# Whole pieces on TensorE in the layer tiles, and an earlier start of the first expert slot

## The chip, the core and the metric

One core of a Trainium2 chip runs the whole program in one launch. The metric is device time in microseconds (us); a run is compared with others of the same kernel on the same kind of core.

## The reference, cut to what matters

The program computes three layers on 4 x 768 = 3072 tokens with 8 heads of 48.

1. A scan with complex decay: for each head `S = a * S + k v^T` and `y = q S` (real part), with `a` scaled to a magnitude of at most 0.999.
2. `h = x @ w_in` (384 to 1024), `solu = h * softmax(h)`, a layer norm of it with the gain `g_ln`, and `x2 = ln @ w_out` (1024 to 384).
3. A mixture of 8 experts: noisy logits `x2 @ w_gate + log(1 + exp(x2 @ w_noise)) * noise`, the two best experts per token with softmax weights, and `out = sum w * (relu(x2 @ w1[e]) @ w2[e])`.

All in float32; the larger products are split into a high and a low part in a rounded float32 form (`F32R`) and made of three matmuls (high-high, high-low, low-high).

## The kernel before, in words

**First phase.** The scan is done in tiles of 128 tokens of one batch entry: T = 24 tiles, six chunks c of four batch entries b, so tile n has `c = n // 4`, `b = n % 4`. Each engine runs its own `body(c, b, n)` for n = 0 to 28, and the body is a software pipeline over tiles: `m = n - 1` (scores, state, output y of the scan), `i = n - 2` (w_in and solu), `j = n - 3` (w_out, logits), `g_ = n - 4` (gate). Order within an engine is the order of the code; engines meet at semaphores.

TensorE's body (`body` under `@block.tensor`) has: turns of kp (L1310); the first 12 of 24 w_in matmuls of tile i (`hidden`, L1345); the scores of tile m (L1367) in four pieces, with the other w_in matmuls between them; the state products (L1402) in eight pieces with three matmuls of w_out (`result`, L1381) behind each; the output y (wide products L1420, at products L1422) with the turns of x2 (`turn_result`) in its middle; the ranks of a finished group (L1439, L1441); the logits (L1449); the turns of z. Scores and the turned z share banks 2 and 3 of PSUM, so the scores wait until zh and zl (ScalarE L748, VectorE L1087) have read them.

ScalarE copies the scores to `at` (L784), GpSimd masks it (L590), and only then may the at products start. ScalarE's body copies `at` before the exponential of tile i (L794) and before the copy of the result to x2 (L809). In a body with b = 0 it also does the logarithms of the next chunk's decays (`squares`, `logs`), in b = 3 the squares and inverses. GpSimd's body has, in order, the mask, a sum `zsum` (L536), the decay of the state (L561 to L566), the sends of tags (L575), rstd (L605, L608), and in b = 0 a second `zsum`, which ScalarE's `scale` (L696) waits for ahead of the next body's zh. VectorE's body has zl, the gate, the maximum of h (nmax, L1161), the softmax product, the state sum, the decay products for k and q (kp, qp) and, in the gaps and in b = 1 to 3, the 107 steps of cumulative products of the next chunk (`fill`); in b = 3 also the Newton steps (L1012, L1016).

The gate works on groups of tiles (`GROUPS`). When a group's last logits are there, VectorE picks the two best (`picked`), TensorE ranks them (in the same body), VectorE makes positions in the next body, and GpSimd sends one tag row per token and expert to a list in memory (`tags`), two sends a tile.

**Passage.** After the last body VectorE works out which expert and which rows of the list each of 31 slots has (14 steps, `slot_step`). SyncE waits for that, loads w1 of slot 0, waits for the end of the first phase, loads the slot's tags (`mine`, L481), w2 and more tags. GpSimd waits for the end of the first phase, clears `xg`, and gathers the slot's rows of x2 into it (L633). ScalarE and VectorE split w1 (L843, L1254) and w2 (L848, L1260) into high and low parts. `raw1`, `raw2` and the split weights lie in memory that the first phase used.

**Second phase.** 31 slots of 256 rows; in each, eight blocks of 9 hidden matmuls (L1319) and 6 result matmuls (L1505), with the next slot's weights split beside them.

The functions that the change touches, and what calls them:

## Time and profile before

| | us |
|---|---|
| median of 3 runs | 1279.58 |
| lowest, highest | 1276.28, 1289.06 |
| the profiled execution | 1290.96 |
| its span (first to last instruction) | 1289.2 |
| busy: TensorE, VectorE, ScalarE, GpSimd | 1126.5, 876.4, 620.8, 446.0 |

The profiled execution is one run; its time is the span and what lies around it. TensorE is busy 87% of the span. A busy share is a mean over stages that have different limits, so the stages have to be read one by one: a window gives the busy time of each engine in a stretch, and PEclk the mean clock granted to TensorE (1.0 is 2.4 GHz, 0.5 is 1.2 GHz). A timeline row has start, duration, engine, line and what it writes and reads, and in brackets how long the engine stood idle before it and what released it.

### The profile page before, as it was taken

How to read it: one execution, taken by the hardware profiler on the slowest of the kernel's cores; microseconds unless marked ns; L12 is line 12 of the kernel's file. 1: busy time of each engine (PE TensorE's matmuls, PEld its weight loads, DVE VectorE, ACT ScalarE, POOL GpSimd, SP SyncE). 2: the span in 40 equal slices, each digit the busy share in tenths (PEclk: the TensorE clock that was granted, in tenths of full speed). 3: DMA queues.
4: the chain of work that ended last, by engine and by line, in shares of the span. 5: the costliest groups of instructions: out<-in, count | busy, mean ns of one | idle time of the engine just before them, and what ended most of it. 6: DMA issues, size and time to landing. Idle time of an engine off the chain costs nothing.

```text
span 1289.2 us, 21867 instructions
## 1 busy us (share of the span) xinstructions
PE 1126.5 (87%) x7864; PEld 977.8 (76%) x7864; DVE 876.4 (68%) x1715; ACT 620.8 (48%) x964; POOL 446.0 (35%) x416
## 2 busy tenths in 40 slices
PE   0048899899989989999994399999999999999996
PEld 0035676676766767667783399999999999999996
DVE  6798579738858946975532476776776776776772
ACT  6422653643573454354432355555555555555551
POOL 3200231233342332223332324444444444444431
PEclk9978899869999969999996599999999999999998
DMA  9411211120031010111100766766776766676740
GB/s 263 135 55 36 53 66 41 49 77 26 26 102 42 25 44 25 42 47 33 49 19 13 245 211 224 253 235 227 243 244 234 264 232 227 236 236 217 241 159 1
DMA packets 85979, 167.50 MB, mean 130 GB/s; under 512 B 18566, under 2 KB 57696, under 8 KB 85872
## 3 DMA queue, kind: packets, MB, share of 16 engines
q1 hardware_dynamic: 72432, 137.71, 33.6%
q0 software_dynamic: 13440, 28.40, 6.2%
q8 instruction: 63, 1.03, 0.4%
q14 instruction: 44, 0.36, 0.1%
HBM read 148.83 MB, written 21.92 MB: 132 GB/s over the span
## 4 chain that ended last, share of the span: by engine, by line
PE 81%; DVE 4%; issue 3%; ACT 2%; DMA 1%; POOL 1%; SPq 0%; POOLq 0%; DVEq 0%; ACTq 0%
PE bank L1319 21%; PE bank L1505 20%; PE bank L1345 11%; PE bank L1381 11%; PE bank L1367 5%; PE bank L1310 5%; PE bank L1420 3%; PE bank L1402 3%; PE bank L1422 2%; DVE turn L1012 1%; PE bank L1449 1%; DVE zl L1087 1%; DVE qp L1040 0%; ACT z L812 0%; DMA mine<-tags 0%
## 5 line engine op out<-in xcount | busy, mean ns | idle before, releaser
L867 ACT ACTIVATE hh<-bank 128x256 fp32r<-128x256 f32 x248 | 95.3, 384 | 253.7 <-PE bank L1319 253.7
L1319 PE MATMUL bank<-sxh,w1h 128*128 128x256 f32 x744 | 212.2, 285 | 1.9 <-DVE sxl L1265 1.9
L1319 PE MATMUL bank<-sxh,w1l 128*128 128x256 f32 x744 | 210.5, 283 | 0.0
L1319 PE MATMUL bank<-sxl,w1h 128*128 128x256 f32 x744 | 210.2, 282 | 0.0
L1288 DVE SCALAR_TENSOR_TENSOR hl<-bank,hh 128x256 fp32r<-128x256 f32 x248 | 104.8, 423 | 117.2 <-ACT hh L867 117.2
L654 POOL DMA_INDIRECT out<-yo,mine x62 | 77.9, 1257 | 276.4 <-DVE yo L1281 267.0
L1505 PE MATMUL bank<-w2h,hh 128*128 128x384 f32 x496 | 167.3, 337 | 0.0
L1505 PE MATMUL bank<-w2l,hh 128*128 128x384 f32 x496 | 166.7, 336 | 0.0
L1505 PE MATMUL bank<-w2h,hl 128*128 128x384 f32 x496 | 166.4, 335 | 0.0
L1319 PEld LDWEIGHTS bank<-sxh,w1h 128*128 128x128 f32 x744 | 140.6, 189 | 2.3 <-DVE sxl L1265 2.3
L1319 PEld LDWEIGHTS bank<-sxh,w1l 128*128 128x128 f32 x744 | 141.7, 190 | 0.0
L1319 PEld LDWEIGHTS bank<-sxl,w1h 128*128 128x128 f32 x744 | 141.1, 190 | 0.0
L1260 DVE TENSOR_TENSOR w2l<-raw,w2h 128x768 fp32r<-128x768 f32 x124 | 118.5, 958 | 27.8 <-ACT w2h L848 27.8
L1254 DVE TENSOR_TENSOR w1l<-raw,w1h 128x1024 fp32r<-128x1024 f32 x93 | 113.5, 1222 | 28.9 <-ACT w1h L843 25.4
L590 POOL TENSOR_SCALAR_AFFINE_SELECT at<-at 128x1024 f32<-128x1024 f32 x24 | 27.6, 1149 | 299.6 <-ACT at L784 299.6
L843 ACT ACTIVATE w1h<-raw 128x1024 fp32r<-128x1024 f32 x93 | 97.6, 1052 | 22.2 <-DMA raw<-in_w 22.2
L848 ACT ACTIVATE w2h<-raw 128x768 fp32r<-128x768 f32 x124 | 103.5, 837 | 0.0
L784 ACT ACTIVATE at<-bank 128x1024 f32<-128x1024 f32 x24 | 24.6, 1024 | 160.6 <-PE bank L1367 160.6
L633 POOL DMA_INDIRECT xg<-xs,mine x62 | 87.8, 1416 | 29.7 <-issue 16.5
L1367 PEld LDWEIGHTS bank<-qp,kp 64*128 64x128 f32 x768 | 56.1, 204 | 53.4 <-issue 53.4
L1345 PE MATMUL bank<-wi_hi,xh 112*128 112x512 f32 x192 | 83.6, 435 | 14.5 <-issue 12.7
L1505 PEld LDWEIGHTS bank<-w2h,hh 128*128 128x128 f32 x496 | 94.3, 190 | 0.2 <-DVE hl L1288 0.2
(183 smaller groups left out, 2553.7 us busy)
## 6 DMA issues: line engine op xcount, KB each, us to landing
raw<-in_w SPq DMA_DIRECT2D x62, 1536.0 KB, 7.0
ar<-in_a_re SPq DMA_DIRECT2D x6, 768.0 KB, 4.5
turn<-in_a_im SPq DMA_DIRECT2D x6, 768.0 KB, 5.8
qk<-in_q SPq DMA_DIRECT2D x48, 96.0 KB, 2.4
qk<-in_k SPq DMA_DIRECT2D x48, 96.0 KB, 2.5
out<-wide SPq DMA_DIRECT2D x9, 512.0 KB, 12.2
vt<-in_v SPq DMA_DIRECT2D x24, 192.0 KB, 2.7
xs<-x SPq DMA_DIRECT2D x24, 192.0 KB, 2.7
```

What stands on the lines that cost most here:

```text
L633: nc.gpsimd.indirect_dma_start(xg[par][:, u, :], None, xs, bass.IndirectOffsetOnAxis(ap=mine[k][:, u, 0:1], axis=0), bounds_check=NTOK - 1 ...
L843: nc.scalar.activation(w1h[par][:, cc, :], raw1[:, cc, :], ACT.Copy).then_inc(w1_hi, 1)
L848: nc.scalar.activation(w2h[par][:, W2C * j:W2C * (j + 1), :], raw2[:, W2C * j:W2C * (j + 1), :], ACT.Copy).then_inc(w2_hi, 1)
L867: nc.scalar.activation(hh[:, f % NH, :], bank[:, f % 2, 0:CAP], ACT.Relu).then_inc(hh_done, 1)
L1254: V.tensor_tensor(w1l[par][:, cc, :], raw1[:, cc, :], w1h[par][:, cc, :].bitcast(F32), ALU.subtract).then_inc(w1_lo, 1)
L1260: V.tensor_tensor(w2l[par][:, cut, :], raw2[:, cut, :], w2h[par][:, cut, :].bitcast(F32), ALU.subtract).then_inc(w2_lo, 1)
L1288: V.scalar_tensor_tensor(out=hl[:, f % NH, :], in0=bank[:, f % 2, 0:CAP], scalar=0.0, in1=hh[:, f % NH, :].bitcast(F32), op0=ALU.max, op1= ...
L1319: ins = MM(dst, stationary[a_](cc), moving[b_](cc), start=(n_ == 0), stop=(n_ == len(terms) - 1))
L1345: ins = MM(bank[:, 4 + half, :], (xh, xl)[a_][0:PR, cc, :], (wi_hi, wi_lo)[b_][0:PR, cc, 512 * half:512 * half + 512], start=(k_ % (3 * NP ...
L1367: ins = MM(bank[:, 2 + h_, p_ * P:(p_ + 1) * P], kp[r_, s, p_, :], qp[r_, s, p_, :], start=(s == 0), stop=(s == 1))
L1381: ins = MM(bank[:, 0, 0:DM], (zh, zl)[a_][:, cc, :], (wo_hi, wo_lo)[b_][:, cc, :], start=(k_ == 0), stop=(k_ == len(x_terms) - 1))
L1505: ins = MM(bank[:, Y_BANK[par] + u, 0:DM], a_[:, f % NH, rows], b_[par][:, f, :], start=(f == 0 and k_ == 0), stop=(f == FC - 1 and k_ == 2))
```

## The change

- **TensorE's tile.** All 24 w_in matmuls stand together; then the 24 result matmuls; then all 16 score matmuls; all state products; all wide products; `turn_result`, which now also waits for the copy of the scores (`a_evac`); all at products. The mask (`at_done`) is waited for only ahead of the at products.
- **ScalarE's tile.** The copy of the scores moves from ahead of the exponential to behind the copy of the result.
- **Gate.** The last groups have 2, 1 and 1 tiles instead of 3 and 1. In bodies behind tile 24 the gate comes ahead of zl, softplus ahead of zh, ranks ahead of the result, and positions in the same body as the ranks; the sends follow one body earlier.
- **Slot 0.** Its expert is always expert 0 and its tags the first 256 rows. SyncE loads w1[0] and w2[0] in body 24, once the decay memory is free (`prepared`); ScalarE and VectorE split w1 in body 25 and w2 in body 26. The tags of slot 0 are loaded as soon as all tags are sent. `mine` and `xg` have memory of their own; GpSimd clears `xg` at the start and makes the tables for the slot list in body 24, where the first threshold becomes -1, so that expert 0 has a slot even if it is empty.

The core of the diff:

```diff
-GROUPS = ((0, 4), (4, 4), (8, 4), (12, 4), (16, 4), (20, 3), (23, 1))
+GROUPS = ((0, 4), (4, 4), (8, 4), (12, 4), (16, 4), (20, 2), (22, 1), (23, 1))
 GROUP_ENDING = {first + count - 1: (k_, first, count) for k_, (first, count) in enumerate(GROUPS)}
...
         cnt = keep("cnt", [P, 4, E])
+        mine = [keep(f"mine{i}", [P, SUB, 2], U32) for i in range(NM)]
+        xg = [keep(f"xg{i}", [P, SUB, DM]) for i in range(2)]
...
+        def prepared(eng):
+
+            eng.wait_ge(m_step, ENDS * (C - 1))
+            eng.wait_ge(rc_done, 2 * C)
+            eng.wait_ge(qp_done, 2 * T)
+            eng.wait_ge(kp_done, 2 * T)
...
+                if n == T:
+                    prepared(sp)
+                    sp.dma_start(raw1[:], w1[0:1].rearrange("e (c p) f -> p (e c) f", p=P)).then_inc(raw1_loaded, 16)
+                    sp.dma_start(raw2[:], w2[0:1].rearrange("e (c p) d -> p (e c) d", p=P)).then_inc(raw2_loaded, 16)
...
+            tags_sent(sp)
+            sp.dma_start(mine[0][:].rearrange("p s i -> p (s i)"),
+                         tags[0:CAP].rearrange("(p s) i -> p (s i)", s=SUB)).then_inc(mine_loaded[0], 16)
             sp.wait_ge(slot_step, 14)
-            load_w1(0)
+            load_mine(1, 1)
             first_phase_over(sp)
-            load_mine(0, 0)
-            load_w2(0)
-            load_mine(1, 1)
             load_mine(2, 2)
 
...
-            SENDS.update({T: (16, 17), T + 1: (18, 19), T + 3: (20, 21, 22), T + 4: (23,)})
+            SENDS.update({T: (16, 17), T + 1: (18, 19, 20, 21), T + 2: (22,), T + 3: (23,)})
...
+                if n == T:
+                    prepared(pool)
+                    nc.gpsimd.iota(slot_no[:], [[1, SLOTS], [0, E]], base=0, channel_multiplier=0,
+                                   allow_small_or_imprecise_dtypes=True).then_inc(tables_ready, 1)
+                    nc.gpsimd.iota(thresh[:], [[0, E], [CAP, MAXS]], base=0, channel_multiplier=0,
+                                   allow_small_or_imprecise_dtypes=True).then_inc(tables_ready, 1)
+                    pool.wait_ge(tables_ready, 2)
+                    nc.gpsimd.memset(thresh[:, :, 0:1], -1.0).then_inc(tables_ready, 1)
...
-            pool.wait_ge(m_step, ENDS * (C - 1))
-            pool.wait_ge(rc_done, 2 * C)
-            pool.wait_ge(kp_done, 2 * T)
-            nc.gpsimd.iota(slot_no[:], [[1, SLOTS], [0, E]], base=0, channel_multiplier=0,
-                           allow_small_or_imprecise_dtypes=True).then_inc(tables_ready, 1)
-            nc.gpsimd.iota(thresh[:], [[0, E], [CAP, MAXS]], base=0, channel_multiplier=0,
-                           allow_small_or_imprecise_dtypes=True).then_inc(tables_ready, 1)
-            first_phase_over(pool)
-            for x in xg:
-                nc.gpsimd.memset(x[:], 0.0).then_inc(xg_ready, 1)
-            pool.wait_ge(xg_ready, 2)
...
+            for s_ in x_sent:
+                pool.wait_ge(s_, 16 * T // 2)
+            pool.wait_ge(xg_ready, 2)
             gather(0, 0, 0)
             gather(1, 1, 1)
+            first_phase_over(pool)
...
+                if n <= T:
+                    softplus(g_)
+                elif n == T + 1:
+                    for cc in range(KC):
+                        w1_piece(0, 0, cc)
+                elif n == T + 2:
+                    for k_ in range(W2P):
+                        w2_piece(0, 0, k_)
...
-                if has(m):
-                    act.wait_ge(a_mm, m + 1)
-                    wait(act, y_mm, m)
-                    nc.scalar.activation(at[:].rearrange("p a n t -> p (a n t)"),
-                                         bank[:, 2:4, :].rearrange("p b x -> p (b x)"), ACT.Copy).then_inc(a_evac, 1)
...
+                if has(m):
+                    act.wait_ge(a_mm, m + 1)
+                    wait(act, y_mm, m)
+                    nc.scalar.activation(at[:].rearrange("p a n t -> p (a n t)"),
+                                         bank[:, 2:4, :].rearrange("p b x -> p (b x)"), ACT.Copy).then_inc(a_evac, 1)
...
+                if n > T:
+                    softplus(g_)
...
+                if n == T + 1:
+                    for cc in range(KC):
+                        w1_piece(0, 0, cc)
+                if n > T:
+                    positions(g_)
+                if n == T + 2:
+                    for k_ in range(W2P):
+                        w2_piece(0, 0, k_)
+
+                if n <= T + 1:
+                    positions(g_ - 1)
...
+                if n <= T:
+                    gate()
...
-                    hidden(0, 3 * NP)
+                    hidden(0, 6 * NP)
+                if n > T:
+                    ranked(g_, LIVE, min(g_ + 1, T))
+                if has(j):
+                    pe.wait_ge(zt_lo, j + 1)
+                    wait(pe, kt_evac, min(m + 1, LIVE))
+                    wait(pe, x2_evac, j)
+                    x_terms = [(cc, a_, b_) for cc in range(FC) for a_, b_ in ((0, 0), (0, 1), (1, 0))]
+                    for k_, (cc, a_, b_) in enumerate(x_terms):
+                        ins = MM(bank[:, 0, 0:DM], (zh, zl)[a_][:, cc, :], (wo_hi, wo_lo)[b_][:, cc, :],
+                                 start=(k_ == 0), stop=(k_ == len(x_terms) - 1))
+                    ins.then_inc(x2_mm, 1)
...
-                        if p_ == NP - 1:
-                            ins.then_inc(a_mm, 1)
-                        else:
-                            hidden(3 * NP + NP * p_, 3 * NP + NP * (p_ + 1))
-                else:
-                    hidden(3 * NP, 6 * NP)
...
+                    ins.then_inc(a_mm, 1)
...
-                            if (s, p_) == (1, NP - 1):
-                                ins.then_inc(w_mm, 1)
-                            k_ = s * NP + p_
-                            result(3 * FC * k_ // (2 * NP), 3 * FC * (k_ + 1) // (2 * NP))
-                else:
-                    result(0, 3 * FC)
+                    ins.then_inc(w_mm, 1)
...
-                    pe.wait_ge(at_done, m + 1)
                     pe.wait_ge(v_loaded, 16 * (m + 1))
                     pe.wait_ge(zero_ready, 4)
                     wait(pe, wide_done, 2 * (m - B + 1))
                     wait(pe, xt_lo, m)
+                    cols = [slice(p_ * P, (p_ + 1) * P) for p_ in range(NP)]
                     for p_ in range(NP):
-                        cols = slice(p_ * P, (p_ + 1) * P)
                         for s in range(2):
-                            MM(bank[0:PR, 7, cols], wide[:, s, p_, 0:PR], qp[:, s, p_, :], start=(s == 0), stop=False)
+                            MM(bank[0:PR, 7, cols[p_]], wide[:, s, p_, 0:PR], qp[:, s, p_, :], start=(p_ == 0 and s == 0), stop=False)
+                    if has(j):
+                        turn_result(j)
+                    pe.wait_ge(at_done, m + 1)
+                    for p_ in range(NP):
                         for h_ in range(2):
-                            ins = MM(bank[64 * h_:64 * h_ + D, 7, cols], vt[:, 2 * p_ + h_, :], at[:, h_, p_, :],
-                                     start=False, stop=True)
-                        if p_ == 1 and has(j):
-                            turn_result(j)
+                            ins = MM(bank[64 * h_:64 * h_ + D, 7, cols[p_]], vt[:, 2 * p_ + h_, :], at[:, h_, p_, :],
+                                     start=False, stop=(p_ == NP - 1))
                     ins.then_inc(y_mm, 1)
...
+                if n <= T:
+                    ranked(g_, min(m + 1, LIVE), min(j, T))
...
+                    if n > T:
+                        wait(pe, pos_step, 5 * ended(g_))
...
@@ -1459,6 +1501,7 @@
             def turn_result(j):
 
                 pe.wait_ge(x2_evac, j + 1)
+                pe.wait_ge(a_evac, min(j + 3, T))
```

## Rows read from the trace of the kernel before

**Rows 1.** Windows by stage: us, busy us of each engine, PEclk, DMA share, GB/s.

```profile
139.50:564.70 425.20, 400.42 (x2747) 292.40 (x2745) 315.90 (x744) 214.26 (x316) 132.26 (x136) 0.92 0.17 48
353.38:454.08 100.70, 94.86 (x689) 69.57 (x688) 79.64 (x188) 53.55 (x80) 34.99 (x36) 0.98 0.19 54
564.70:666.01 101.31, 99.44 (x697) 77.74 (x696) 49.85 (x115) 41.91 (x66) 32.77 (x39) 1.00 0.17 44
666.01:730.84 64.83, 26.34 (x132) 23.52 (x130) 20.18 (x72) 14.13 (x24) 20.76 (x24) 0.67 0.24 81
730.84:1289.20 558.36, 547.04 (x3900) 545.49 (x3900) 381.65 (x554) 291.53 (x491) 234.27 (x181) 0.99 0.65 218
```

**Rows 2.** Windows of two boundary tiles (b = 0), columns as above.

```profile
353.38:381.38 28.00, 24.47 (x172) 17.82 (x171) 16.06 (x29) 19.44 (x27) 11.92 (x11) 0.94 0.38 107
454.08:491.94 37.86, 34.33 (x172) 24.44 (x171) 16.05 (x29) 19.54 (x27) 13.45 (x12) 0.64 0.16 37
```

**Rows 3.** TensorE's timeline at two boundaries: start, us, line, count, idle before, releaser.

```profile
362.27 0.72 PE L1367 MATMUL bank<-qp,kp 64*128 64x128 f32 x8 [3.53 <-DVE zl L1087]
...
462.97 1.23 PE L1367 MATMUL bank<-qp,kp 64*128 64x128 f32 x8 [3.53 <-DVE zl L1087]
```

**Rows 4.** TensorE's timeline of one tile (b = 2), columns as above.

```profile
408.24 0.47 PE L1345 MATMUL bank<-wi_hi,xh 112*128 112x512 f32 x1 [1.28 <-issue]
...
411.15 0.72 PE L1367 MATMUL bank<-qp,kp 64*128 64x128 f32 x8
...
417.15 0.29 PE L1402 MATMUL bank<-vt,kt 128*48 128x48 f32 x4
...
424.66 0.60 PE L1420 MATMUL bank<-qp,wide 128*112 128x128 f32 x4
```

**Rows 5.** Chain of waits in the last tiles: start, us, what, count.

```profile
600.06 4.37 PE bank L1381 x24
...
667.78 5.51 PE bank L1345 x24
```

**Rows 6.** VectorE's timeline, b = 0 to b = 3 of one block.

```profile
369.20 1.23 DVE L1161 TENSOR_REDUCE nmax<-bank 128x1 f32<-128x1024 f32 x1 [4.93 <-PE bank L1345]
...
385.02 1.23 DVE L1087 TENSOR_TENSOR zl<-bank,zh 128x1024 fp32r<-128x1024 f32 x1 [0.58 <-ACT zh L748]
...
392.16 1.23 DVE L1161 TENSOR_REDUCE nmax<-bank 128x1 f32<-128x1024 f32 x1 [2.30 <-PE bank L1345]
...
416.60 1.23 DVE L1161 TENSOR_REDUCE nmax<-bank 128x1 f32<-128x1024 f32 x1 [1.53 <-PE bank L1345]
...
454.33 0.69 DVE L1204 TENSOR_TENSOR xl<-bank,xh 112x512 fp32r<-112x512 f32 x1 [2.45 <-ACT xh L828]
```

**Rows 7.** ScalarE's timeline in the boundary tile.

```profile
369.87 1.02 ACT L784 ACTIVATE at<-bank 128x1024 f32<-128x1024 f32 x1 [5.12 <-PE bank L1367]
...
370.80 1.11 ACT L794 ACTIVATE z<-bank,nmax 128x1024 f32<-128x1024 f32 x1
...
371.88 0.94 ACT L686 ACTIVATE cum<-cum,tiny 128x768 f32<-128x768 f32 x1
```

**Rows 8.** GpSimd's timeline at the end of the boundary tile.

```profile
380.56 0.19 POOL L605 TENSOR_SCALAR rstd<-mv 128x1 f32<-128x1 f32 x1 [1.40 <-ACT bank L815]
...
381.39 1.81 POOL L536 TENSOR_TENSOR cum<-cum 128x768 f32<-128x768 f32 x1
```

**Rows 9.** GpSimd's timeline in the tail.

```profile
707.14 0.96 POOL L575 DMA_INDIRECT tags<-tag,idx  x1 [0.31 <-issue]
...
710.98 1.42 POOL L626 MEMSET xg<- 128x768 f32 x2 [2.10 <-DMA tags<-tag,idx]
```

**Rows 10.** Chain of waits in the tail.

```profile
715.81 5.08 DMA mine<-tags
```

**Rows 11.** VectorE's timeline in the tail.

```profile
673.31 1.23 DVE L1161 TENSOR_REDUCE nmax<-bank 128x1 f32<-128x1024 f32 x1 [3.22 <-PE bank L1345]
...
721.95 1.23 DVE L1254 TENSOR_TENSOR w1l<-raw,w1h 128x1024 fp32r<-128x1024 f32 x1 [8.71 <-ACT w1h L843]
```

More of the change, by code:

```diff
@@ L200, in solu_moe_program @@
         prev = [m2(f"prev{i}", [P, SUB, DM]) for i in range(2)]
-        mine = [m2(f"mine{i}", [P, SUB, 2], U32) for i in range(NM)]
         bank = psum("bank", [P, 8, 512])
@@ L521, in _ @@
                 nc.gpsimd.memset(md[:, NG], 1.0).then_inc(gaps_ready, 1)
+            for x in xg:
+                nc.gpsimd.memset(x[:], 0.0).then_inc(xg_ready, 1)
             pool.wait_ge(const_ready, 7)
@@ L737, in _, with softplus @@
             nc.scalar.activation(wo_hi[:], raw_out[:], ACT.Copy).then_inc(w_hi_ready, 1)
+            def softplus(g_):
+                group, first, count = GROUP_ENDING.get(g_, (None, 0, 0))
+                from_ = B - count
+                if group is not None:
+                    act.wait_ge(lg_copy, g_ + 1)
+                    wait(act, gate_step, gated(group))
+                    nc.scalar.activation(spl[:, 0, from_:], lg[:, from_:, E:2 * E], ACT.Exp).then_inc(sp_done, 1)
+                    act.wait_ge(sp_done, 2 * group + 1)
+                    nc.scalar.activation(spl[:, 1, from_:], spl[:, 0, from_:], ACT.Ln, bias=1.0).then_inc(sp_done, 1)
             def body(c, b, n):
@@ L1060, in _, with positions @@
             newton(1)
-            def body(c, b, n):
-                m, i, j, g_ = n - 1, n - 2, n - 3, n - 4
-                has = lambda t: 0 <= t < T
-                prep = c + 1 < C
-                share = PRODUCTS[b] if prep else 0
-                made = [PRODUCTS[b - 1] if prep and b else 0]
-                def fill(count=1):
-                    for k_ in range(made[0], min(share, made[0] + count)):
-                        product_op(c + 1, k_)
-                        made[0] = k_ + 1
-                if has(g_):
-                    dve.wait_ge(lg_mm, g_ + 1)
-                    group, first, count = GROUP_ENDING[min(t for t in GROUP_ENDING if t >= g_)]
-                    wait(dve, sp_done, 2 * group)
-                    wait(dve, gate_step, gated(group))
-                    V.tensor_copy(lg[:, B - count + g_ - first], bank[:, 6, DM:DM + 2 * E]).then_inc(lg_copy, 1)
-                if has(j):
-                    dve.wait_ge(zt_hi, j + 1)
-                    wait(dve, x2_mm, j)
-                    V.tensor_tensor(zl[:].rearrange("p c t -> p (c t)"), bank[:, 2:4, :].rearrange("p b x -> p (b x)"),
-                                    zh[:].rearrange("p c t -> p (c t)").bitcast(F32), ALU.subtract).then_inc(zt_lo, 1)
-                group, first, count = GROUP_ENDING.get(g_ - 1, (None, 0, 0))
+            def positions(t_):
+                group, first, count = GROUP_ENDING.get(t_, (None, 0, 0))
                 from_ = B - count
@@ L1323, in _, with ranked @@
             pe.wait_ge(const_ready, 9)
+            def ranked(g_, added, copied):
+                group, first, count = GROUP_ENDING.get(g_, (None, 0, 0))
+                if group is not None:
+                    pe.wait_ge(gate_step, gated(group + 1))
+                    wait(pe, w_added, added)
+                    wait(pe, lg_copy, copied)
+                    wait(pe, pos_step, 5 * group)
+                    pe.wait_ge(picked_ready, 1)
+                    ranks = bank[:, 6, DM + 2 * E:DM + 2 * E + (B + 1) * E].rearrange("p (t e) -> p t e", e=E)
+                    from_ = B - count
+                    MM(ranks[:, from_:], causal[:], picked[:, from_:], start=True, stop=False)
+                    for t in range(from_, B):
+                        ins = MM(ranks[:, t + 1:], ones[:], picked[:, t:t + 1].to_broadcast([P, B - t, E]), start=False,
+                                 stop=(t == B - 1))
+                    ins.then_inc(rank_mm, 1)
             def body(c, b, n):
@@ L1428, in body @@
                     turn_result(j)
-                group, first, count = GROUP_ENDING.get(g_, (None, 0, 0))
-                if group is not None:
-                    pe.wait_ge(gate_step, gated(group + 1))
-                    wait(pe, w_added, min(m + 1, LIVE))
-                    wait(pe, lg_copy, min(j, T))
-                    wait(pe, pos_step, 5 * group)
-                    pe.wait_ge(picked_ready, 1)
-                    ranks = bank[:, 6, DM + 2 * E:DM + 2 * E + (B + 1) * E].rearrange("p (t e) -> p t e", e=E)
-                    from_ = B - count
-                    MM(ranks[:, from_:], causal[:], picked[:, from_:], start=True, stop=False)
-                    for t in range(from_, B):
-                        ins = MM(ranks[:, t + 1:], ones[:], picked[:, t:t + 1].to_broadcast([P, B - t, E]), start=False,
-                                 stop=(t == B - 1))
-                    ins.then_inc(rank_mm, 1)
+                if n <= T:
+                    ranked(g_, min(m + 1, LIVE), min(j, T))
                 if has(j):
                     pe.wait_ge(x2t_evac, j + 1)
+                    if n > T:
+                        wait(pe, pos_step, 5 * ended(g_))
                     wait(pe, w_added, min(m + 1, LIVE))
```

171 lines of the change are left out of this document (87 added, 84 removed).

## The prediction

> **What bounds the kernel now.** I read the windows by stage first, then TensorE's timeline of one tile, then the queues behind each wait that is left. The profiled execution took 1290.96 us, its span is 1289.2, and 1.76 lie around it; the median of three runs is 1279.58, 11.4 less. In the windows [rows 1] sixteen tiles in four blocks of four take 425.20 us; five more, 101.31; the passage to the experts, 64.83, with TensorE busy for only 26.34 of them; the experts, 558.36 with TensorE busy for 547.04. The last stretch has the same loops before and after the change, and I leave it as it is.
>
> A block costs 100.70 us where the granted clock hardly falls [rows 1], so 4 x 100.70 = 402.8 and 22.4 of the 425.2 belong to the clock. How, [rows 2] show: the same boundary tile (b = 0) takes 28.00 us at a mean clock of 0.94 and 37.86 at 0.64, much of it at 1.2 instead of 2.4 GHz. Both have the same stall before the scores, 3.53 us for zl [rows 3]. After such a stall the clock falls, once for a moment and once for about a tile; the long fall costs 9.9 us. The runs differ by 12.8 us, about one such fall, so the median probably has one fewer than the profile.
>
> **The pieces.** On TensorE the block from the first w_in matmul to the first state product is 417.15 - 408.24 = 8.91 us, the one of result and state products 424.66 - 417.15 = 7.51 [rows 4]. Unbroken, 24 w_in matmuls took 5.51 us and 24 result matmuls 4.37 in the last tiles [rows 5]. For 16 score matmuls (two records each) the interleaved form gives 4 x 0.65 = 2.6; with the switches gone I take 2.1 (x8 in 0.72 less one latency of about 0.3 leaves 0.06 per record). State products: 8 x 0.24 = 1.9 interleaved, about 1.4 unbroken, by the same reasoning. So 8.91 becomes 7.6 and 7.51 becomes 5.8: 3.0 us of TensorE less per tile with state products, 1.3 without. Bounds: nothing (all switches cost what they did) and 3.9 (if the output pieces, now all wide ones before all at ones, gain too).
>
> **What the pieces are worth in a block.** TensorE's 3.0 us do not come through directly, since VectorE is busy for 79.64 of 100.70 [rows 1] and GpSimd's queue has a chain of its own. By tile:
> - b = 0. zl is late for reasons that stay (the Newton pair of the previous tile). It is now needed after 24 w_in matmuls and no longer after 12, so the stall of 3.53 shrinks by about half of 5.51, less 1.1 by which w_in itself can start earlier: about 1.9 remain. Behind it the scores come last, and ScalarE copies them after the exponential, four logarithm steps and the result copy. VectorE sat 4.93 us before nmax, which takes 1.23 [rows 6], so nmax can run from 364.3 to 365.7, the exponential (1.11 [rows 7]) to 366.9, four logarithm steps (0.94 the first [rows 7], 3.5 together) to 370.4, the result copy of about 0.5 to 370.9. There the at copy starts, where it was 369.87 [rows 7]: 1.0 late. From it GpSimd runs the mask, one zsum, three decay steps, two sends, rstd and the second zsum, ending 381.39 + 1.81 = 383.20; in this chain only the wait of 1.40 for var can go [rows 8]. The second zsum thus ends 0.4 earlier, and with it the scaling, zh and zl of the next tile. That is all that b = 0 yields, although TensorE could be about 5 us faster.
> - b = 1. From zl (385.02 [rows 6]) VectorE's work stays; its wait of 2.30 before nmax [rows 6] goes, as h is complete before VectorE asks. 2.3 us.
> - b = 2. The same wait, 1.53 [rows 6], goes. 1.5 us.
> - b = 3. xl waited 2.45 for ScalarE [rows 6]. The result comes early enough for ScalarE to copy it without a wait; the at copy of 1.02 [rows 7] has moved into the row behind it. 2.45 - 1.02 = 1.4 us.
> Sum 0.4 + 2.3 + 1.5 + 1.4 = 5.6 us a block, 22.5 for four. Bounds: nothing, if GpSimd's row slips by more than 1 us; 11.4, if GpSimd's chain could move too (the full 3.0 in three tiles and 5 in b = 0 less what VectorE's own work forbids). I take 5.6, since each term is a wait that has a row.
>
> A place where page and sum meet: GpSimd's 4 us of mask and decay now fall on other VectorE operations. No row here shows that overlap for these operations, and I count zero; the bounds are nothing better and 4 us a block worse, VectorE standing for all of GpSimd's time in the tile that paces. The Trainium skill (GPSIMD Engine Reference, Specifications) says that GpSimd's SBUF interface contends with VectorE instructions that have two SBUF inputs; by it a shift onto the decay products of k and q would lengthen them, and the sum would lose a part of that bound.
>
> **Tiles 20 to 24** (101.31 us). The first is a boundary without logarithms: 1.9 of stall, and the pieces, 2.5: 4.4. Its four followers fill TensorE, which loses 1.3 minus a wait of about 0.2 for the mask, now right behind scores, state and wide products: 1.1 each. Together -9; bounds -3 and -12.
>
> **The clock.** 22.4 us are lost in the profile. Afterwards the stall at b = 0 is halved, but TensorE is further ahead of VectorE, which is the working above read the other way: in b = 1 it reaches zl, which comes only 0.4 earlier, with all 24 w_in matmuls done and stands there about 3 us, and each tile whose VectorE work sets its length leaves TensorE its 3.0 less what the tile shrinks, standing before kp and xl: about 2 to 4 more in b = 1, 3 in b = 2. The likeliest is one long fall, 10 us; so -12.
>
> **The tail.** Removed from the way: six of the eight sends behind the last ranks. The last of the eight started at 707.14, and its landing released GpSimd at 710.98 [rows 9]. With the last tile alone in its group and 20 to 22 sent before, the last send starts two sends of about 1.27 after the tags are ready (the pause before a first send and the steps of VectorE included, about 703.4): -3.7. Slot 0's tags no longer wait for the slot list and the weights: issued 4.83 after the landing (715.81 - 710.98, [rows 9, 10]), now about 0.5: -4.3. Their landing, 5.08 [rows 10], was beside two weight transfers; I take 3.5, -1.6, with 0 and -2.6 as bounds. The gather of xs and what follows are as before. The weights of slot 0 are split 50 us early, on memory free once the last q and k products are done; the loads go ahead of SyncE's send of tile 21, which waits for x2 anyway, and the issue costs it under 1 us. Added to the way: in body 25 VectorE does gate(21), three w1 pieces of 1.23 [rows 11] and positions(21) ahead of nmax, which started at 673.31 [rows 11]; it will start at about 676, and everything down to the last logits moves by 2.8. The next gate and ranks ahead of the result cost another 0.1 to 0.4. The w2 pieces lie under 24 result matmuls. GpSimd has the tables and the two memsets done early, hidden by its waits. Sum -3.7 - 4.3 - 1.6 + 2.9 = -6.7, say -7; bounds -3 and -12 (the experts start warmer).
>
> **Sum.** 1290.96 - 22.5 - 9 - 12 - 7 = 1240.5. Against the median the clock term is worth about nothing (one fall there, one here): 1279.58 - 38.5 = 1241.1. I predict 1240.
>
> **Rivals.**
> - *The chain gives way* (17%): GpSimd's row in b = 0 proves shorter and no long fall comes. The block is then bound by VectorE's 79.6 us and its waits, about 90 instead of 95: another 5.2 x 4 = 21, and 10 of clock, 1209 to 1230. For it: TensorE has 3 us a tile less. Against: the 0.4 above.
> - *The clock falls once in every block* (22%). For it: three new places where TensorE stands 3 us, the size of the stall that has brought falls [rows 3]. Four falls instead of one, 10 each: 1270. Against: at 1.2 GHz a lighter tile loses some of it into waits that are there anyway. The Trainium skill (TensorE: Matmul & The Clock Gate, HAM oscillation) describes a loop whose waits bring the fall back in every round. By that rule alone this case would have a third of the chance; the trace has 22.4 us of loss in four blocks, two long falls and a rest, so it has less.
> - *The steps change nothing in the blocks* (12%). The at copy behind the logarithms makes TensorE wait for the mask as long as it saved in switches; only the clock, the last tiles and the tail remain: 1290.96 - 12 - 9 - 7 = 1263.
> - *Slower* (8%): the same waits bring the fall twice in a block, ahead of the result in b = 1 and ahead of w_in in b = 2. Price 9.9 each [rows 2]; from the forecast without falls, 1230, five make 1280, six 1289 and eight 1309. It decides from five on. Against: short falls are also seen, and VectorE's bound hides part of a slow TensorE.
> - *Forecast* 41%: 1230 to 1252.
>
> **Numbers.** 1% is what a measurement tells from no change: 1266.8 and 1292.4 are the bounds. Faster: forecast, the first rival, the third (nearly all) and some of the second: 0.77. Within 1%: most of the second and a part of the others, 0.16. Slower 0.07. The range 1210 to 1270 holds the forecast, the third, most of the first and half of the second.
>
> **What would show it.** L1381 in runs of 24 taking about 4.4 us; a stall of about 1.9 before the result at b = 0 and a new one of about 3 at b = 1; no VectorE wait before nmax in b = 1 and b = 2; blocks of 95 us where the clock is 1.0; the second zsum of b = 0 at the end of the same row of GpSimd work; tags released with two sends behind the last ranks; the first expert matmul about 7 us nearer to body 24's logits. Wrong would be: blocks under 91 (GpSimd did not bind) or over 100 (the mask does), a mean clock under 0.85 in all four, or a wait for at before L1422 of more than 1 us in b = 2.

## The result, and the profile after

The changed kernel takes 1225.15 us (median of 4 runs, 1223.89 to 1225.62); the kernel before, beside it, 1282.55 (1276.28 to 1289.06). The ratio is 0.955, with a 95% interval of 0.950 to 0.960. The profiled execution took 1223.89 us against 1290.96, which is 67.1 less, and every term below is measured between these two. The profiled execution of the kernel before lies 8 us above its median, that of the kernel after 1 us under its own, so a part of the 67.1 is the choice of the execution.

The windows by stage of the kernel after, cut at the same places as those of before [rows 1]: the logits matmul of bodies 3, 19 and 24, and the first expert matmul. Columns are the same.

```profile
0.00:134.21 134.21, 46.60 (x396) 39.79 (x396) 107.63 (x231) 58.40 (x69) 26.75 (x39) 0.90 0.40 118
134.21:520.19 385.98, 335.92 (x2746) 294.01 (x2745) 326.13 (x745) 215.02 (x317) 149.03 (x133) 0.91 0.20 52
520.19:612.59 92.40, 88.54 (x698) 78.85 (x697) 49.44 (x116) 42.28 (x68) 36.87 (x41) 0.98 0.35 82
612.59:664.45 51.86, 26.88 (x132) 23.72 (x133) 25.35 (x89) 16.24 (x29) 25.04 (x25) 0.72 0.14 46
664.45:1222.20 557.75, 546.35 (x3900) 544.79 (x3900) 378.02 (x550) 289.59 (x488) 233.06 (x181) 0.99 0.64 218
```

The four blocks are 39.2 us shorter (385.98 against 425.20), tiles 20 to 24 by 8.9, the passage to the experts by 13.0, the start by 5.3, the experts by 0.6. In the blocks TensorE is now idle for 385.98 - 335.92 = 50 us (24.8 before), so it has stopped setting the pace.

One block of the kernel after, by tile (b = 0 to b = 3), same columns:

```profile
326.37:347.95 21.58, 18.87 (x171) 16.59 (x170) 16.09 (x28) 20.32 (x29) 12.85 (x10) 1.00 0.39 89
347.95:374.40 26.45, 21.84 (x170) 19.03 (x170) 20.00 (x42) 12.19 (x18) 14.34 (x15) 0.87 0.24 72
374.40:398.75 24.35, 22.84 (x169) 19.54 (x169) 21.40 (x54) 8.14 (x12) 4.48 (x6) 0.79 0.12 33
398.75:424.13 25.38, 21.67 (x181) 18.96 (x180) 24.72 (x68) 13.12 (x22) 8.45 (x9) 0.93 0.11 32
```

Before, the tiles of the undisturbed block took 28.00 [rows 2], 22.94, 24.45 and 25.31 us. The first two together went from 50.94 to 48.03; the last two did not move (49.76, 49.73). The cut at the logits moves time between neighbours, since those of b = 0 now come earlier, which shortens b = 0 and lengthens b = 1 (26.45 against 22.94); so the two are read together. In b = 3 VectorE is busy for 24.72 of 25.38 us.

The pieces, in the chain of waits of the kernel after (start, us, what, count), where before the w_in and result matmuls stood between scores and state products [rows 4]:

```profile
602.62 4.17 PE bank L1430 x24
606.79 2.10 PE bank L1444 x32
608.89 0.02 issue
608.92 1.02 ACT at L855
```

The result takes 4.17 us (4.37 in [rows 5]) and the scores 2.10, which is the 2.1 of the sum.

### The profile page after: what moved, and what is told of

It is laid out like the page before. It is cut to its first block, busy times and chain, and to the rows that moved or that the text cites. A ratio compares the mean times of both kernels' runs of the same rounds, so it can differ in the third digit from the quotient of the medians.

```text
span 1222.2 us, 21907 instructions
## 1 busy us (share of the span) xinstructions
PE 1044.3 (85%) x7866; PEld 981.2 (80%) x7866; DVE 886.6 (73%) x1729; ACT 621.5 (51%) x967; POOL 470.8 (39%) x417
## 4 chain that ended last, share of the span: by engine, by line
PE 55%; issue 2%; ACT 1%; DVE 1%; DMA 1%; POOL 0%; POOLq 0%; DVEq 0%; ACTq 0%; SPq 0%
PE bank L1367 22%; PE bank L1548 21%; PE bank L1411 3%; PE bank L1430 3%; PE bank L1358 3%; PE bank L1444 1%; PE bank L1491 1%; PE bank L1477 0%; ACT at L855 0%; PE bank L1471 0%; DMA xg<-xs,mine 0%; DMA tags<-tag,idx 0%; PE bank L1387 0%; POOL at L612 0%; ACT z L859 0%
## 5 line engine op out<-in xcount | busy, mean ns | idle before, releaser
L1411 PE MATMUL bank<-wi_hi,xh 112*128 112x512 f32 x192 | 86.8, 452 | 25.2 <-issue 22.8
L1358 PE MATMUL bank<-ident,kp 128*128 128x128 f32 x160 | 28.0, 333 | 80.9 <-DVE kp L1081 80.8
L651 POOL DMA_INDIRECT xg<-xs,mine x62 | 86.2, 1390 | 24.6 <-issue 16.8
L1548 PEld LDWEIGHTS bank<-w2l,hh 128*128 128x128 f32 x496 | 94.3, 190 | 0.0
```

Source lines behind the costliest of these rows:

```text
L651: nc.gpsimd.indirect_dma_start(xg[par][:, u, :], None, xs, bass.IndirectOffsetOnAxis(ap=mine[k][:, u, 0:1], axis=0), bounds_check=NTOK - 1 ...
L1358: ins = nc.tensor.transpose(out_, in_, ident[:])
L1411: ins = MM(bank[:, 4 + half, :], (xh, xl)[a_][0:PR, cc, :], (wi_hi, wi_lo)[b_][0:PR, cc, 512 * half:512 * half + 512], start=(k_ % (3 * NP ...
L1548: ins = MM(bank[:, Y_BANK[par] + u, 0:DM], a_[:, f % NH, rows], b_[par][:, f, :], start=(f == 0 and k_ == 0), stop=(f == FC - 1 and k_ == 2))
```

## The experiments

All windows below have the columns of [rows 1]. The median of the kernel before lay between 1282.6 and 1289.8 us from one series to the next; each ratio is against the runs beside it. The stages of all kernels, in us, cut where the rows above are cut, come from one profiled execution each (that of the kernel before took 1290.96):

| kernel | to body 3 | bodies 4 to 19 | bodies 20 to 24 | to first expert matmul | median |
|---|---|---|---|---|---|
| before | 139.50 | 425.20 | 101.31 | 64.83 | 1282.6 |
| after | 134.21 | 385.98 | 92.40 | 51.86 | 1225.2 |
| e1 pieces alone | 134.83 | 384.01 | 94.06 | 62.78 | 1238.0 |
| e2 TensorE order alone | 141.31 | 426.03 | 116.76 | 66.78 | 1311.3 |
| e3 groups 3, 1 | 134.29 | 385.97 | 92.68 | 50.73 | 1223.7 |
| e4 decay first | 134.49 | 376.00 | 91.13 | 52.42 | 1215.5 |
| e5 no decay | 134.33 | 360.80 | 93.64 | 53.98 | 1201.5 |
| e6 filler in before | 140.71 | 406.38 | 111.16 | 65.03 | 1282.5 |
| e7 filler in after | 134.47 | 416.74 | 95.91 | 51.94 | 1258.4 |
| e8 weights in flight | 135.22 | 385.34 | 94.14 | 59.30 | 1231.1 |
| e9 short filler | 140.76 | 399.67 | 101.32 | 64.59 | 1267.9 |
| e10 e3 and e4 | 134.28 | 375.85 | 91.26 | 49.76 | 1212.4 |
| e11 before, no decay | 139.37 | 397.10 | 104.34 | 64.27 | 1266.1 |

**The pieces alone.** The kernel before with TensorE's new order and the at copy behind x2 on ScalarE; groups and slot 0 as before.

```diff
-                    hidden(0, 3 * NP)
+                    hidden(0, 6 * NP)
+                if has(j):
...
+                    x_terms = [(cc, a_, b_) for cc in range(FC) for a_, b_ in ((0, 0), (0, 1), (1, 0))]
+                    for k_, (cc, a_, b_) in enumerate(x_terms):
...
                     nc.scalar.activation(x2[par][:], ...)
+                if has(m):
+                    act.wait_ge(a_mm, m + 1)
...
```

> The kernel before with the tile change alone: TensorE's order in unbroken pieces and the copy of the scores behind the result copy; groups, slot 0 and the passage as before. The changed kernel saved 66 us of span, of which its windows put 51 to 53 ahead of the tail (5 at the start, 39 in the four blocks, 9 in tiles 20 to 24) and 13 in the tail. If the two parts are independent, this run is at 1236 to 1240. Rival: part of the blocks' gain comes from the shifted memory or from chance in the clock; then it lies above 1250.

1237.95 us, ratio 0.9625 (0.956 to 0.969), in the first range. Its blocks (384.01 us) are those of the changed kernel, and its start is within 0.6 us of it. What bodies 0 to 19 gained, and 7.3 of the 8.9 in tiles 20 to 24, is the order's; slot 0, the groups and the earlier sends have the rest: 1.7 there and 10.9 in the passage.

**TensorE's order without ScalarE's move.** As e1, without the last edit of its diff: the at copy stays ahead of the exponential.

> As the run before, but the copy of the scores stays ahead of the exponential on ScalarE. The scores now come last on TensorE, so the copy waits for them and holds up the exponential of tile i, in b = 0 the logarithms, and the copy of the result. If ScalarE's order was needed, each tile grows by about the 3 to 4 us by which the exponential moves back less what VectorE's own bound hides: 1280 to 1310. Rival: VectorE and GpSimd pace the tiles anyway, and the move is worth nothing: 1236 to 1242.

1311.33 us, ratio 1.019 (1.011 to 1.026): slower than before by 1 to 3%, and 1 us above the expected range. ScalarE's timeline of one tile of it:

```profile
421.97 1.02 ACT L784 ACTIVATE at<-bank 128x1024 f32<-128x1024 f32 x1 [11.24 <-PE bank L1376]
423.02 1.11 ACT L794 ACTIVATE z<-bank,nmax 128x1024 f32<-128x1024 f32 x1
...
427.77 1.15 ACT L812 ACTIVATE z<-z,mv 128x1024 f32<-128x1024 f32 x1 [3.07 <-DVE mv L1186]
```

ScalarE stands 11.24 us for scores that TensorE now makes last, and the exponential, queued behind the copy, starts only at 423.02; z, x2t and the logits follow it. The copy's move by one place on ScalarE is worth 73 us between e2 and e1: in the profiles 42 in the blocks, 23 in tiles 20 to 24 and 10 in the other stages. The pieces and that move are one change.

**The old groups.** The changed kernel with groups of 3 and 1 for tiles 20 to 23, the sends of the three still a body earlier than before.

```diff
-GROUPS = (... (16, 4), (20, 2), (22, 1), (23, 1))
+GROUPS = (... (16, 4), (20, 3), (23, 1))
-  T + 1: (18, 19, 20, 21), T + 2: (22,), T + 3: (23,)
+  T + 1: (18, 19), T + 2: (20, 21, 22), T + 3: (23,)
```

> The changed kernel with the old last groups of 3 and 1 tiles, everything else as changed (gate, positions and sends one body earlier). My prediction gave 3.7 us to the six sends taken from behind the last ranks and put that on the groups; by it this run is at 1228 to 1230. Rival: the earlier body did it, the six sends of tiles 20 to 22 end before the last ranks anyway, and without gate(21) and positions(21) ahead of nmax the last tile is even 1 to 3 us earlier: 1222 to 1226.

1223.71 us (1222.55 to 1224.16), the range of the rival. It is 1.4 below the changed kernel, whose runs it overlaps (1223.89 to 1225.62), so the third group bought nothing; in the profiles its extra positions cost about 1 us (50.73 against 51.86 to the first expert matmul). Two sends stand behind the last ranks here too. What took six of eight out of the way is the body in which they are sent.

**Decay first, and no decay.** Theory 1: the last two tiles of a block gained nothing because GpSimd's mask and decay now run beside VectorE's products and lengthen them. Theory 2: the overlap costs wherever it is put. e4 puts the decay ahead of the mask; e5 goes without it.

```diff
+                if B <= n < T:
+                    decay_state(n)
                 if has(m):
...
-                if B <= n < T:
-                    decay_state(n)
```

In e5 three operations on one element stand for the decay:

```diff
-                nc.gpsimd.tensor_tensor(st2[:], state[:, b], ...)
+                nc.gpsimd.memset(st2[one_], 0.0).then_inc(state_step, 1)
...
```

> The changed kernel with GpSimd's three decay steps of the state ahead of the mask instead of behind it. Theory 1: tiles b = 2 and b = 3 did not shrink because mask and decay now run beside VectorE's k products (kp 1.09 us on average instead of 0.69) and these are on the path to kp and xl, and the boundary tile is paced by GpSimd's chain, which gets 3.6 us shorter: blocks lose 3 to 5 us each, 1205 to 1213. Theory 2: VectorE's total sets the length, and the contention only moves to its cumulative products: 1221 to 1227.

> The changed kernel without the three decay steps on GpSimd (three one-element operations keep their places; the state is not decayed, so this part of the computation is left out). It prices all that the steps cost where they stand now: 2.7 us of GpSimd a tile and their overlap with VectorE's k products. Theory 1 (the place behind the mask is the trouble): the run ahead of this one, with the steps ahead of the mask, already has nearly all of it, so 1208 to 1215. Theory 2 (any overlap with VectorE costs the same): clearly lower than that run's 1215.5, 1195 to 1207.

e4: 1215.52 us (1213.74 to 1219.22), ratio 0.946, outside both ranges. e5: 1201.53 (1200.97 to 1202.32), ratio 0.935, in the range of theory 2. Both theories hold in part: without decay the blocks lose 25.2 us, of which the other place gives back 10.0. The windows of the blocks of e4 and e5, beside the 385.98 of the kernel after above:

```profile
134.49:510.49 376.00, 324.00 (x2747) 284.15 (x2745) 320.78 (x745) 214.06 (x316) 140.51 (x135) 0.95 0.19 54
134.33:495.13 360.80, 317.57 (x2746) 278.99 (x2745) 303.79 (x745) 214.05 (x316) 101.86 (x134) 0.97 0.21 56
```

e5 takes away all that the decay costs: its overlap with VectorE, its length in GpSimd's row and whatever the clock regains (0.97 against 0.91). The overlap is by far the largest: the same 745 VectorE operations are busy for 326.13 us with the decay and 303.79 without, 22.3 of the 25.2. The place where it happens, in VectorE's and GpSimd's timelines of the kernel after at the end of b = 2:

```profile
398.38 2.56 DVE L1081 TENSOR_TENSOR kp<-cum,qk 128x512 f32<-128x512 f32 x2
```

```profile
396.99 1.01 POOL L583 TENSOR_TENSOR st<-state,md 128x384 f32<-128x384 f32 x1
397.96 1.02 POOL L585 TENSOR_TENSOR st<-state,md 128x384 f32<-128x384 f32 x1
399.07 1.33 POOL L588 TENSOR_TENSOR state<-st,st 128x384 f32<-128x384 f32 x1
```

The pair of k products takes 2.56 us beside the decay. It takes 1.29 where the decay is not beside it (VectorE's timelines of e4):

```profile
439.96 1.29 DVE L1081 TENSOR_TENSOR kp<-cum,qk 128x512 f32<-128x512 f32 x2
```

Small operations show it more sharply. VectorE's timeline of the kernel after in b = 1, and the three decay operations on GpSimd, from 369.55 to 372.48:

```profile
369.82 0.88 DVE L965 TENSOR_TENSOR ct<-cum,ar 128x192 f32<-128x192 f32 x1
370.63 0.99 DVE L970 TENSOR_TENSOR ct<-cum,turn 128x192 f32<-128x192 f32 x1
371.66 1.04 DVE L973 TENSOR_TENSOR cum<-ct,ct 128x192 f32<-128x192 f32 x1
372.74 0.36 DVE L965 TENSOR_TENSOR ct<-cum,ar 128x192 f32<-128x192 f32 x1
```

```profile
369.55 0.94 POOL L583 TENSOR_TENSOR st<-state,md 128x384 f32<-128x384 f32 x1
370.46 0.96 POOL L585 TENSOR_TENSOR st<-state,md 128x384 f32<-128x384 f32 x1
371.49 0.99 POOL L588 TENSOR_TENSOR state<-st,st 128x384 f32<-128x384 f32 x1
```

The same form takes 0.36 us alone and 0.88 to 1.04, about the length of one GpSimd operation, beside the decay. Each of the three products ends 0.20 to 0.22 us behind the GpSimd operation beside it (370.70 behind 370.49, 371.62 behind 371.42, 372.70 behind 372.48). And kp's delay reaches TensorE: its turns of kp wait for the pair, and xl, which stands seven steps of the cumulative products (3.5 us) behind kp on VectorE, ends at 405.07 and lets b = 3's w_in start (kernel after):

```profile
401.00 1.09 PE L1358 MATMUL bank<-ident,kp 128*128 128x128 f32 x8 [0.48 <-DVE kp L1081]
...
404.39 0.68 DVE L1267 TENSOR_TENSOR xl<-bank,xh 112x512 fp32r<-112x512 f32 x1
...
405.17 0.47 PE L1411 MATMUL bank<-wi_hi,xh 112*128 112x512 f32 x1 [3.08 <-issue]
```

The stall of 3.08 us is not itself the price: in e4 TensorE stands 3.14 at this place.

**Was it there before?** The kernel before with the edit of e5.

> The kernel before without GpSimd's three decay operations of a tile (a one-element operation in place of each, so the state isn't decayed). Theory 1 (beside the decay VectorE's products were no bound in the old order, where TensorE paced and the products ran at 0.69 us; the price is new in the changed order): under 5 us, 1275 to 1288. Theory 2 (the decay costs what it costs in any order, 24 us in the changed kernel): 1255 to 1265.

1266.07 us, ratio 0.983 (0.978 to 0.988), 1 us above the range of theory 2; but the total misleads, since no long fall of the clock is in this trace. By tile, at 22.94 (b = 1), 22.95 (b = 2) and 24.27 (b = 3) against 22.94, 24.45 and 25.31, the decay costs 2.5 us a block in the old order; b = 0 is left out, since the clock differs there. In the new order it is 25.2 / 4 = 6.3. The overlap itself was there before. The window of e11's blocks:

```profile
139.37:536.47 397.10, 381.90 (x2747) 281.00 (x2745) 300.46 (x744) 214.28 (x316) 93.63 (x136) 0.97 0.18 51
```

VectorE is busy for 300.46 us instead of 315.90 [rows 1], so the decay lengthened its operations by 15.4 us in the old order and by 22.3 in the new one. What changed more is how much of it counts: some 10 us in four blocks before, nearly all of it after, since VectorE now sets the pace. One of its places before, VectorE's timelines of the kernel before and of e11 at the same operation:

```profile
419.96 0.94 DVE L938 TENSOR_TENSOR ct<-cum,turn 128x192 f32<-128x192 f32 x1
```

```profile
404.41 0.36 DVE L937 TENSOR_TENSOR ct<-cum,turn 128x192 f32<-128x192 f32 x1
```

**The clock, by filling the stall.** e6 puts 30 matmuls of constants, into a bank that is free then, into the stall of b = 0 [rows 3] in every fourth body from body 4; e9 puts 17 there in bodies 4, 8, 12 and 16 alone.

```diff
+            def warm(count, at0):
+                for _ in range(count):
+                    MM(bank[0:PR, at0, 0:64], ident[:, 0:PR], ones[:, 0:64], start=True, stop=True)
...
                 if has(j):
+                    if n in (4, 8, 12, 16):
+                        warm(17, 5)
                     pe.wait_ge(zt_lo, j + 1)
```

> The kernel before with 30 small matmuls of constants, written to an idle bank and overwritten, in the wait for zl of each boundary tile (b = 0, from tile 4 on). Where the 3.53 us of standing bring the clock down, this keeps it up. If the 22.4 us that the profile lost in the four blocks hang on that stall, 1260 to 1268 with a clock of 1.0 behind each boundary; if the falls come from elsewhere or the matmuls themselves are in the way, 1280 to 1292.

> The kernel before with 17 constant matmuls (about 3.4 us) in TensorE's stall ahead of the reversed copy's last correction, in bodies 4, 8, 12 and 16 alone; with 30 of them in every fourth body the clock stayed full from 124 to 673 us and 18.8 us came back between bodies 3 and 19, but 9.9 us were lost in bodies 20 and 24, where no stall of that length was. Theory 1 (the two long falls of the clock cost 20 us, and filling the stall alone removes them): stage of bodies 4 to 19 at 394 to 400 us instead of 425, bodies 20 to 24 as before, time 1260 to 1266. Theory 2 (the falls cost little, and the longer fill hid something else): 1275 to 1285. If 3.4 us of filler do not hold the clock, a long fall is in the trace again and the time is as before's.

e6: 1282.53 us, ratio 0.997 (0.995 to 0.999), outside the first range and in the second. Its windows of bodies 4 to 19 and 20 to 24:

```profile
140.71:547.09 406.38, 396.79 (x2987) 298.63 (x2985) 318.58 (x744) 214.28 (x316) 132.45 (x136) 1.00 0.17 50
547.09:658.25 111.16, 111.16 (x818) 89.84 (x817) 49.83 (x115) 41.92 (x66) 32.78 (x39) 1.00 0.16 40
```

The clock stayed full and 18.8 us came back in the blocks; the filler took 6.02 us where the stall was 3.53, and bodies 20 and 24 paid 9.9 for filler in a stall that they don't have at that length. e9, cut to the stall (3.46 us), took 1267.92 us (1266.34 to 1272.53), ratio 0.985 (0.980 to 0.990), 2 us above the range of theory 1, with the stage of bodies 4 to 19 in it:

```profile
140.76:540.43 399.67, 388.50 (x2883) 289.39 (x2881) 316.53 (x744) 214.36 (x316) 132.42 (x136) 1.00 0.18 51
342.07:368.49 26.42, 26.29 (x205) 20.33 (x204) 16.05 (x29) 19.45 (x27) 11.93 (x11) 1.00 0.39 114
```

At full clock b = 0 takes 26.42 us instead of 28.00 or 37.86 [rows 2], although zl comes as late: the falls of the profiled execution cost 425.20 - 399.67 = 25.5 us, 11.4 each long one. The Trainium skill (TensorE: Matmul & The Clock Gate, HAM oscillation) counts half of the time at the lower level as lost. 64.8 us at that level lie in these blocks of the trace, so an estimate by that page is 32; e9 measured 25.5, and the measurement stands.

**The same in the changed kernel.** Filler of 10 to 36 such matmuls in TensorE's waits before zl and xl, in bodies 4 to 20.

```diff
+                    wait(pe, var_done, i)
+                    if B <= n < T - 3:
+                        warm({0: 0, 1: 10, 2: 36, 3: 36}[b], 4)
                     pe.wait_ge(xt_lo, i + 1)
-                    wait(pe, var_done, i)
...
                 if has(j):
+                    if b < 2 and B <= n < T - 3:
+                        warm(24, 7)
                     pe.wait_ge(zt_lo, j + 1)
```

> The changed kernel with small matmuls of constants in TensorE's waits: 24 ahead of the result in b = 0 and 1, 10 to 36 ahead of w_in in b = 1 to 3, for tiles 4 to 19. The changed kernel has 13 short falls there, but TensorE is not what paces the tiles. If so, the clock goes up and the time stays: 1222 to 1228. Rival: a slow TensorE lengthens h, the scores and the output on the chain, and 1 us a fall comes back: 1208 to 1216.

1258.36 us (1256.0 to 1265.3), 33 above the changed kernel and outside both ranges:

```profile
134.47:551.21 416.74, 407.68 (x3787) 376.73 (x3785) 329.67 (x745) 216.60 (x317) 148.98 (x133) 0.99 0.19 49
```

TensorE is busy for 407.68 of 416.74: the filler exceeded the waits and became the bound. It says nothing on what the remaining short falls cost, which stays open.

**Weights in flight.** The changed kernel with slot 0's weights (3 MB) loaded once more, unused, ahead of the last tags.

```diff
+            sp.wait_ge(pos_step, 5 * len(GROUPS))
+            sp.dma_start(raw1[:], w1[0:1] ...)
+            sp.dma_start(raw2[:], w2[0:1] ...)
             tags_sent(sp)
             sp.dma_start(mine[0] ...
```

> The changed kernel with slot 0's w1 and w2 (3 MB) loaded a second time just ahead of the last tags and of slot 0's tag load, as they were in flight there before. The tail gave 13 us where I had 7; the landings of tags, slot tags and gathered rows were 1.2, 3.5 and 1.0 us shorter than before. If the weights in flight made them long, this run loses 3 to 6 us: 1228 to 1231. Rival: the landings are short because of the static address or the idle queue: 1224 to 1226.

1231.13 us (1228.65 to 1233.38), at the upper end of the first range. The three landings of the chain of waits behind the last logits, first in the kernel after, then in e8:

```profile
651.04 2.60 DMA tags<-tag,idx
653.70 1.58 DMA mine<-tags
...
657.55 3.18 DMA xg<-xs,mine
```

```profile
653.37 6.58 DMA tags<-tag,idx
...
660.01 2.45 DMA mine<-tags
...
664.74 5.55 DMA xg<-xs,mine
```

7.36 us became 14.58, so weights in flight lengthen small landings. But e8 does not put them where the kernel before had them. Windows over the last tags and the slot tags, first of the kernel before, then of e8 (the last two columns are DMA share and GB/s):

```profile
707.14:710.98 3.84, 0.00 (x0) 0.00 (x0) 1.79 (x7) 0.00 (x0) 1.73 (x3) 0.50 0.05 3
715.81:720.89 5.08, 0.00 (x0) 0.00 (x0) 0.00 (x0) 0.13 (x1) 0.00 (x0) 0.50 0.95 354
```

```profile
653.37:659.95 6.58, 0.00 (x0) 0.00 (x0) 1.50 (x8) 0.00 (x0) 0.96 (x1) 0.50 1.04 378
660.01:662.46 2.45, 0.00 (x0) 0.00 (x0) 0.00 (x0) 0.00 (x0) 0.00 (x0) 0.50 0.52 155
```

Before, the last tags landed with next to nothing in flight, and the slot tags beside the weights; in e8 it is the other way round, and the slot tags come when the load is nearly over. Over its gather e8 moves 261 GB/s, the kernel after 146. So e8 shows the mechanism; it does not measure its share in the 13.0 of the passage. The fall of the slot tags' landing from 5.08 to 1.58 fits it. The 1.2 by which the last tags landed sooner does not: neither kernel had weights in flight there, and in e4 and e5, which have the tail of the kernel after, that landing took 2.57 and 3.83 us, so its length varies by as much from one profile to the next.

From the last logits to the first expert matmul it is 21.38 us after and 35.51 in e1. Of these 14.1 us, 4.2 are the sends (the last one starts 12.22 behind the logits in e1, 7.97 after) and 3.5 the landing of the slot tags (5.04 to 1.58).

**The best of these together.** Decay first and groups 3, 1.

> The kernel after with the decay ahead of the mask on GpSimd (1215.5 on its own) and groups 3 and 1 (1223.7 against 1225.2 on their own). If the two add up: 1212 to 1216, kp at 0.75 us mean. If the groups' 1.1 us in the tail were chance: 1215 to 1217.

1212.41 us (1210.45 to 1216.76, 6 runs), ratio 0.942 (0.938 to 0.946), in the range for adding up, though its runs overlap those of e4 (1213.74 to 1219.22). The passage took 49.76 us against 52.42 in e4. It beats both kernels.

## Why the prediction was right, and which terms were not

The direction and the range (1210 to 1270) held, and the steps worked by the means foreseen: shorter pieces, fewer losses to the clock, an earlier first slot. The time is 15 us under the 1240 of the sum and outside the forecast's own 1230 to 1252. That it is not further off is in part luck: the pieces gave less than their term, and the clock, the tail and the start gave more. Term by term, of the profiled 67.1:

- **The pieces in the blocks: -22.5 predicted, -16.8 measured** (402.8 to 385.98), or -13.7 if the line of full clock is e9's 399.67 and not four times a block that still had one short fall. Against e9, b = 0 and b = 1 gave 10.5 us in the four blocks (10.8 predicted; 6.3 of them in the first block), b = 2 gave 4.3 (6.0 predicted) and b = 3 lost 1.1 (a gain of 5.6 predicted). The step that failed is the one where the overlap of GpSimd's mask and decay with VectorE's products was counted at zero, with 4 us a block as its bound. e5 gives the decay 25.2 us in four blocks, 6.3 a block; 22.3 of them are VectorE operations made longer, and 10.0 are a matter of place (e4). The step says that no row shows this overlap; the trace of the kernel before has such rows, one of them at 419.96 above. The overlap also kept b = 0's row on GpSimd from getting shorter: the wait of 1.40 for var [rows 8] went, but zsum ran 1.98 and the last two decay steps 1.29 and 1.33, and from the at copy to the end of the second zsum it is 13.34 us where it was 13.33. In the term for the scores, the latency of about 0.3 us stands in no row; the 2.1 that came of it measured 2.10.
- **The clock: -12 predicted, -22.4 by the same cut, -25.5 by e9.** No long fall is left: the longest between bodies 4 and 19 lasts 10.2 us where two lasted 27.3, and there are eleven. The mean there is no better (0.91), but TensorE has slack. That the long falls went in all is not explained by the halved stall alone (see the last section), so this term's size was not reasoned out.
- **Tiles 20 to 24: -9 predicted, -8.9 measured.**
- **The tail: -7 predicted, -13.0 measured.** The parts on the way to the last send (-3.7 predicted, 12.21 to 7.97 is -4.2) and to the slot tags (-4.3, measured -4.8) were right; body 24's part cost 1.6 net instead of 2.9. The added work did cost 3.2 (27.27 in e1, 30.48 after), and the pieces, which this part left out, gave 1.6 back (28.92 to 27.27). Mis-sized were the landings: the slot tags fell from 5.08 [rows 10] to 1.58 us instead of 3.5, beyond the bound of 2.6 set for them, and those of the last tags (-1.2) and the gather (-1.0), counted at zero, fell as well. e8 shows that weights in flight can do this; for the last tags the cause stays open. The total lies outside the bounds of 3 and 12. The -3.7 was put to the groups; e3 shows that it is the earlier body.
- **The start: 0 predicted, -5.3 measured**, by the order (e1 has 4.7 of it). No step was made for bodies 0 to 3, where the same pieces run.

Summed: 16.8 + 22.4 + 8.9 + 13.0 + 5.3 + 0.6 = 67.0.

**The rivals.** The time lies in the interval of "the chain gives way" (1209 to 1230), and one half of it occurred: no long fall came. The other did not: GpSimd's row was not shorter, and blocks took 95.35 to 97.76 us and not 90. "The clock falls once in every block" had the count right and more, and the price wrong: short falls under VectorE's bound and not 9.9 each. "The steps change nothing in the blocks" is excluded by e1, whose blocks (384.01) are under the 399.67 of full clock in the old order. "Slower" found its place elsewhere: in e2, one copy on ScalarE decides between 0.96 and 1.02. Of the marks set for the trace, the stalls before the result are 2.06 and 2.96 us at their longest in b = 0 and b = 1 (about 1.9 and 3 foreseen), but at b = 0 the last two blocks have none; nmax waits no longer in b = 1, but still 1.92 in the b = 2 above, where the clock is 0.79.

## What to carry to other kernels

When one engine's order is tightened, price the others' overlaps anew: an overlap that was mostly hidden while another engine set the pace counts in full once the lengthened engine does (10 of 15.4 us before, 25.2 by e5 after, 22.3 of them the lengthening). Filling a stall of 3.5 us gave back up to 11.4 us of clock behind it (e9), and filler longer than the stall gave nothing in total (e6). And the transfers that can be issued early should be, since what is in flight can lengthen a small landing on the critical path.

## What the hardware showed that was not expected

- A GpSimd operation with SBUF operands does not slow a VectorE product by a share; the product seems to stand until it is over: 0.36 us became 0.88 to 1.04, 1.29 for a pair became 2.56. The Trainium skill (SBUF — State Buffer, SBUF: two separate sides) says so: the shared port pair is an exclusive lock, and a VectorE instruction with two SBUF inputs fully waits for a GpSimd instruction that reads SBUF. The trace agrees: each product ends 0.20 to 0.22 us behind the GpSimd operation beside it. What that comes to in a block depends on which operations meet; here the decay made VectorE's operations 22.3 us longer in sixteen tiles.
- Loads of 3 MB in flight, at 378 GB/s, raised the landing of the last tags from 2.60 to 6.58 us (e8).
- Removing the decay from the kernel before also removed its long clock falls, although the stall of 3.53 us is still there (e11 has four falls of 6.8 us in the blocks, where the kernel before had two of 27.3 and two shorter ones): the long fall does not follow from the stall alone. What else decides stays open.
